# Packing the on-chip tensors of a three-layer kernel more tightly: start addresses on multiples of 64 and 32 bytes in place of 2048

## The reference, cut to what matters

```python
# layer 1, for each block b of 64 tokens
intra = (qb @ kb.T * Dmask) @ vb
inter = (qb * lam_pow) @ kv_state
out[:, :, sl] = intra + inter
kv_state = lam_block * kv_state + (kb * rev_pow).T @ vb
# layer 2, x is the output of layer 1 as (2, 768, 512)
xk = mu_k * x + (1 - mu_k) * x_prev
xr = mu_r * x + (1 - mu_r) * x_prev
k = maximum(xk @ w_k, 0)              # 512 -> 1024
x = sigmoid(xr @ w_r) * (k * k @ w_v)
# layer 3
gate = sigmoid(sum over 5 taps of conv_w[k] * x shifted by k)
return (gate * (x @ w_val)) @ w_out
```

## Time and profile before

| | us |
|---|---|
| median of 3 runs | 283.02 |
| lowest, highest | 282.29, 283.13 |
| the profiled execution, its own time | 283.13 |
| its span in the profile | 281.2 |
| TensorE busy | 272.2 |
| VectorE busy | 168.1 |
| ScalarE busy | 118.7 |
| GpSimd busy | 43.1 |

### The profile page before, as it was taken

The page is one execution under the profiler, slowest core; times in us unless marked ns, Lnnn a source line. Parts: engine busy times, 40 slices in busy tenths (PEclk is TensorE's granted clock), DMA queues, the critical chain, the costliest instruction groups (busy, mean ns, idle before and its releaser), DMA issues.

```text
span 281.2 us, 4245 instructions
## 1 busy us (share of the span) xinstructions
PE 272.2 (97%) x1748; PEld 226.9 (81%) x1748; DVE 168.1 (60%) x253; ACT 118.7 (42%) x197; POOL 43.1 (15%) x36
## 2 busy tenths in 40 slices
PE   8799987999999999999999999999999999999996
PEld 8688766888888888888888888888888888888885
DVE  3859999775868012446696754526987599515000
ACT  2036534757687113437741133567325404522121
POOL 0696696005800000000000000000000000000000
PEclk9999999999999999999999999999999999999999
DMA  7999997000000000000000000170000000300222
GB/s 269 421 372 403 369 417 309 2 0 1 2 0 0 0 2 0 0 0 2 0 0 0 3 0 0 37 265 0 0 0 2 0 0 0 114 37 0 112 77 112
DMA packets 7506, 23.42 MB, mean 83 GB/s; under 512 B 832, under 2 KB 1216, under 8 KB 7488
## 3 DMA queue, kind: packets, MB, share of 16 engines
q1 hardware_dynamic: 7344, 23.07, 21.3%
q10 hardware_dynamic: 144, 0.09, 0.1%
HBM read 20.01 MB, written 3.15 MB: 82 GB/s over the span
## 4 chain that ended last, share of the span: by engine, by line
PE 92%; DMA 4%; DVE 2%; issue 1%; ACT 0%; DVEq 0%
PE ps L652 27%; PE ps L650 27%; PE ps L651 27%; PE ps L715 4%; PE ps L666 3%; DMA qk<-in_qk 2%; PE ps L700 2%; PE ps L683 2%; DMA prm<-in_prm 1%; DVE dec L548 1%; DVE qdec L552 1%; DVE pT L462 0%; ACT x L292 0%; ACT out_sb L368 0%; DVE om L554 0%
## 5 line engine op out<-in xcount | busy, mean ns | idle before, releaser
L650 PE MATMUL ps<-xk_h,wk_h 128*128 128x512 f32 x96 | 37.5, 390 | 0.0
L651 PE MATMUL ps<-xk_l,wk_h 128*128 128x512 f32 x96 | 37.4, 389 | 0.0
L652 PE MATMUL ps<-xk_h,wk_l 128*128 128x512 f32 x96 | 37.3, 389 | 0.0
L650 PE MATMUL ps<-kk_h,wv_h 128*128 128x512 f32 x96 | 37.3, 389 | 0.0
L651 PE MATMUL ps<-kk_l,wv_h 128*128 128x512 f32 x96 | 37.3, 389 | 0.0
L652 PE MATMUL ps<-kk_h,wv_l 128*128 128x512 f32 x96 | 37.3, 389 | 0.0
L501 DVE SCALAR_TENSOR_TENSOR kk_f<-ps,ring 128x512 f32<-128x512 f32 x24 | 16.6, 691 | 30.6 <-ACT ring L321 30.5
L525 DVE SCALAR_TENSOR_TENSOR gate<-x,prm,gate 128x512 f32<-128x512 f32 x48 | 32.6, 746 | 0.0
L321 ACT ACTIVATE ring<-ps 128x512 f32<-128x512 f32 x24 | 14.4, 598 | 32.9 <-PE ps L652 32.9
L338 ACT ACTIVATE gate<-x,prm 128x512 f32<-128x512 f32 x12 | 8.7, 725 | 42.6 <-DVE x L511 42.6
L650 PEld LDWEIGHTS ps<-xk_h,wk_h 128*128 128x128 f32 x96 | 18.0, 188 | 3.9 <-issue 0.2
(11 more groups left out here) (69 smaller groups left out, 518.2 us busy)
## 6 DMA issues: line engine op xcount, KB each, us to landing
qk<-in_qk SPq DMA_DIRECT2D x12, 512.0 KB, 5.5
kv<-in_kv SPq DMA_DIRECT2D x12, 512.0 KB, 6.3
out<-out_sb SPq DMA_DIRECT2D x11, 256.0 KB, 2.0
wk_raw<-in_w_k SPq DMA_DIRECT2D x4, 512.0 KB, 6.9
wv_raw<-in_w_v SPq DMA_DIRECT2D x4, 512.0 KB, 10.9
wr_raw<-in_w_r SPq DMA_DIRECT2D x2, 512.0 KB, 8.0
w_raw<-in_w_val SPq DMA_DIRECT2D x2, 512.0 KB, 4.4
w_raw<-in_w_out SPq DMA_DIRECT2D x2, 512.0 KB, 7.0
```

What stands on the lines that cost most here:

```text
L650: nc.tensor.matmul(to, left(0), right(0), start=(i == 0), stop=False)
L651: nc.tensor.matmul(to, left(0), right(1), start=False, stop=False)
L652: done = nc.tensor.matmul(to, left(1), right(0), start=False, stop=(i == last))
```

## The change

The first address was rounded up to a multiple of 2048 and is now rounded up to a multiple of 64. The region of `x`, 4 * 4 * 1546 = 24,736 bytes, was rounded up to 26,624 and now takes 24,736.

```diff
-        top = [-(-nc.sbuf_base // 2048) * 2048]
+        top = [-(-nc.sbuf_base // 64) * 64]
...
-        x_at = take(-(-4 * KT * XW // (2 * KB)) * 2 * KB)
+        x_at = take(4 * KT * XW)
```

## The result

The changed kernel takes 291.08 us, the median of 4 runs (290.7 to 291.88), against 283.07 us before (282.29 to 283.13, 4 runs). The ratio is 1.0293, with a 95% interval of 1.0263 to 1.0324: slower by about 2.9%. The forecast was no change, 283.1 us with a range of 282.0 to 284.6; it was wrong. The profiled execution of the changed kernel took 289.81 us itself, and what follows is read from it. So the profiles differ by 6.7 us where the medians differ by 8.0; the other executions of the changed kernel lie up to 2.1 us above the profiled one, and no trace shows why.

What follows compares the result with a forecast made beforehand. It took TensorE's undisturbed matmul slots to bound four fifths of the time and several things in turn the attention stage. 283.13 us plus four terms of 0 gave 283.1 us, range 282.0 to 284.6.

Steps and rivals of the forecast that it cites:

- TensorE in the matrix stage: 1020 matmul slots from about 50 us on: start addresses change nothing, 0 taken, bounds -2.1 to +1.2 us.
- The sign that it named for this case: Fewer than 221 matmuls in a stretch of 50 us would show that TensorE's reads pay.
- The first rival: Every slot from 50 us on: TensorE's reads pay for the start, 1 to 3 ns each, 284.1 to 286 us; chance 0.10.
- The 39 ns of cover of the weight load: Matrix stage: weight loads of 188 ns lie under the slot of 227 with 39 ns to spare.
- VectorE, ScalarE, GpSimd: Hidden by TensorE in the matrix stage; GpSimd's 12.2 us run in the attention stage could move -0.1 to +0.1; 0 taken.
- Loads: Transfers of chunks and weights, landing of qk of chunk 9 in the attention stage: 0 taken, bounds 0 and +0.8 us.
- The rule of the Trainium skill that the prediction weighed: Loads: a row starting off a multiple of 256 bytes takes an additional piece; +2.0 us by pieces, +0.4 by beats.
- Rhythm of the attention stage: Overlap of GpSimd's kdec with VectorE may turn: faster, 280.9 us, chance 0.11; slower, +1.6 us at most, chance 0.05.
- the rival: Attention stage falls into a faster rhythm: waits of 1.04, 0.33 and 0.86 us to gain, 2.2 us; chance 0.11.
- prm and stores: Parameter landing, 4.0 us, and last store, 1.7 us: 0.1 us more in each, 0.2 at worst; 0 taken.

Runs made afterwards that it cites:

- e5_three_distances: Kernel before, with xk 128, xr 256 and kk 512 bytes past the 2048 grid and the weights on it; 286.3 us in one run.
- e1_base_only: Changed kernel without its second part: first address a multiple of 64, region of x rounded up to a multiple of 2048 again; 283.49 us, ratio to before 1.0012.
- e8_x_to_256: Changed kernel with the region of x rounded up to a multiple of 256 bytes; 283.81 us, ratio 1.0008.
- e3_all_32: Kernel before with every region moved up by 32 bytes, distances between operands as before; 283.39 us, ratio 1.0015.
- e7_others_160: Kernel before with ring, r, own and prm moved by 160 bytes, which TensorE doesn't read in the matrix stage; 282.99 us, ratio 0.9972.
- the first four experiments: Change without its second part, 283.49 us; without its first, 290.75; kernel before with all regions up 32 bytes, 283.39; with 64 bytes behind x, 286.46.
- the scan: TensorE alone, nothing of the reference: 45 cases of 24 matmuls with operands at chosen distances; 227.5 ns a slot at distance 256, 233 at 224.

## Why the prediction was wrong, point by point

- **TensorE in the matrix stage**: this is the step that failed. It said "I take 0", with -2.1 to +1.2 us as bounds; it came out at +7.43 us. Two things were wrong in it. The bounds were carried over from VectorE's and ScalarE's spread over starts, and these instructions told nothing of TensorE, whose weight loads run beside its matmuls. And the equal weight loads and slots were taken as evidence that starts don't matter, though all of them stand at distances that are multiples of 512: that is one point of the cost, not a range. The rows held no other distance. The text said that no row has TensorE reading from finer starts, but spoke of each operand's start and not of the distance between two, and took 0 all the same; with no row at hand the term had no bound. The sign that it named for this case, fewer than 221 matmuls in 50 us, is what came: 215.
- **The first rival** had the place and the price right: every slot, 1.0 us a nanosecond. Its size, 1 to 3 ns, was too small: 7.6 ns in most slots, 6.6 in `project`. Its mechanism was told as the start of an operand; it is the distance of two, and moving all by 32 bytes costs nothing. It had a chance of 0.10.
- **The 39 ns of cover of the weight load** were read rightly as an amount and wrongly as protection: the weight load still takes 188 ns and the slot still grew.
- **VectorE, ScalarE, GpSimd**: 0, as forecast. Line 525 has 744 ns against 747, and GpSimd's run, 32.75 to 44.97 us before, is 31.89 to 44.20 after: 12.3 us against 12.2.
- **Loads**: the rates are alike, 423 GB/s against 422 from 4 to 8 us. `qk` of chunk 9 landed at 35.54 us, 0.71 later than before, after a transfer that took 7.17 us in place of 6.49. That isn't shown to be the addresses: in e5_three_distances, whose chunks start on multiples of 512, the same transfer took 7.16 us. The landing cost nothing in the end, but not as reckoned. The prediction had `update` wait for `kdec` of chunk 8 in any case; in the changed kernel GpSimd's run begins 0.86 us earlier (31.89 against 32.75), that `kdec` ends at 34.61 + 1.51 = 36.12 us in place of 36.98, before TensorE needs it, and the waits of 1.04 and 0.33 us are gone from the chain. The rule of the Trainium skill that the prediction weighed (DMA: Bandwidth & Descriptors, How a descriptor splits into AXI transactions) would by its count in pieces, 17 in place of 16, have made the landing 2.0 us later; the trace doesn't show that. Its count in beats, +0.4 us, one trace can't tell from nothing.
- **Rhythm of the attention stage**: it does shift. The matrix stage starts at 49.85 us before, at 49.08 after and 49.12 in e1_base_only: 0.77 us earlier, a third of the 2.2 us that the rival held possible. In e8_x_to_256 it starts at 50.48. The granted clock is 1.00 through the attention stage of all four. In e3_all_32 it starts at 50.84 and in e7_others_160 at 51.56, but there the granted clock was 0.50 from 13 to 15 us, where TensorE did 28 and 26 matmuls and the kernel before 50 at 1.00; so their later starts aren't the rhythm alone. From 8 to 12 us TensorE was busy for 1.84 of 4 us in e3_all_32 and for 2.18 in the kernel before, and why the clock fell in one and not in the other stays open. This dip, not the addresses, goes with much of the spread of the runs: of the 19 executions of the kernel before that were made beside the first four experiments, the 8 with a mean clock of 0.999 or more have a median of 282.0 us and the 11 with 0.993 or 0.994 one of 284.2.
- **prm and stores**: 0, as forecast; `prm` lands after 4.04 us against 4.00, the last store again after 1.7 us. The prediction gave the rows of this store 2048 bytes; they have 1024 (128 KB over 128 partitions), and nothing hangs on it.

The parts of the chain of the changed kernel on which this rests:
```profile
0.73 4.04 DMA prm<-in_prm
...
28.37 7.17 DMA qk<-in_qk
...
43.43 0.87 issue
...
49.08 0.43 PE ps L650
```
GpSimd's timeline in the changed kernel, and the stretch from 13 to 15 us in the kernel before and in e3_all_32, in this order:
```profile
31.89 1.53 POOL L241 TENSOR_TENSOR faded<-state,qdec 128x256 f32<-128x256 f32 x1 [0.40 <-DVE state L476]
...
34.61 1.51 POOL L253 TENSOR_TENSOR kdec<-kv,dec 128x512 f32<-128x512 f32 x1
```
```profile
13.00:15.00 2.00, 2.00 (x50) 1.64 (x47) 1.59 (x3) 0.00 (x0) 2.00 (x3) 1.00 1.03 403
```
```profile
13.00:15.00 2.00, 2.00 (x28) 1.66 (x30) 1.15 (x2) 0.00 (x0) 2.00 (x3) 0.50 1.02 403
```

## What to carry to other kernels

Back-to-back matmuls of this shape (128x128 by 128x512), whose slots nothing covers, are fastest when the moving and the stationary operand start at the same residue modulo 256 bytes; which residue makes no difference among those tried, 0, 32, 64, 128 and 160. For other shapes measure first: at 256 moving or 32 stationary columns another distance was faster. A region of an odd size goes last, or its size is rounded up to 256; that costs at most 224 bytes here, where tensors are placed in steps of 32. Read a matmul's start to start, not the duration of one instruction of another engine, and when all rows of a profile stand at one value of what the change varies, the rows bound nothing.

## What the runs showed of the hardware that wasn't expected

- The slot of a 128x128 by 128x512 matmul in fp32r (the type of the high and low parts) depends on the distance between its operands' starts with a period of 256 bytes: 226.7 ns at 0, 228.9 at 64, 233.2 to 234.3 at the other multiples of 32.
- Off the best distance the slots aren't noisy. They repeat a few lengths in a fixed order, 3 at a distance of 64 and 7 at 160, the same in the kernel and with TensorE alone.
- At 256 moving columns the order of preference is another one: 120.0 ns at distance 0 and 117.2 at 160. In this kernel only the 24 last slots have that shape.
- In the scan's first 14 slots, all at distance 0, 13 took 426 or 427 ns, and from the sixteenth on they took 226 to 236. 512 columns at the lower level of the clock, 1.2 GHz, make 426.7 ns, so these slots look like the lower level with nothing on top; the granted clock that the profile gives for 12 to 18 us is 1.00, and so doesn't confirm it. By the same count 512 columns make 213 ns at 2.4 GHz, an estimate, and the best slot has 13 ns on top of that.
- A shift of all four operands by 16 bytes, within a tensor, cost 6.6 ns (233.3), where 64 cost nothing and 160 nothing after some slots; a distance of 508 cost nothing and one of 4 cost 10 ns (236.7); distances of 8, 16, 48 and 80 took 231.1 to 233.3. What steps below 32 do wasn't followed up.
- The Trainium skill (SBUF — State Buffer, Who interferes with whom) gives TensorE two independent read ports, for the moving operand and for weight loads, and says that it waits on no one. As far as other engines go, the runs agree: moving their tensors by 160 bytes cost nothing, and the slots were the same with them idle. For TensorE's own two operands the measured 226.7 and 234.3 ns decide: their distance matters.
